# Attention steps 39 to 41 of the second chunk one step earlier, and seven scalings moved from VectorE to GpSimd

## The chip, the core and the metric

The program runs on one core of one Trainium2 chip. Its time is the device time of one execution in microseconds (us). The engines are named as in the profile: PE (TensorE, with PEld its weight loads), ACT (ScalarE), DVE (VectorE), POOL (GpSimd) and SP (SyncE, which here only issues DMAs). Each runs its own list of instructions in order; they wait for each other through semaphores.

## The reference

Top-32 attention over 4 batches, 8 heads, 576 positions and a head size of 64, then two feed-forward layers over 2304 tokens (512 to 2048 to 512). All data is fp32.

```python
scores = scale * np.matmul(q, k.transpose(0, 1, 3, 2))
kth = np.partition(scores, -top_k, axis=-1)[..., -top_k:-top_k + 1]
scores = np.where(scores >= kth, scores, -1000000000.0)
scores = scores - np.max(scores, axis=-1, keepdims=True)
attn = np.exp(scores)
attn = attn / (np.sum(attn, axis=-1, keepdims=True) + 1e-09)
x = np.matmul(attn, v)            # transposed and reshaped to (2304, 512)
h = x @ w_in                      # layer 0
x = np.maximum(0.01 * h, h) @ w_out
h = x @ w_in2                     # layer 1
g = np.where(h >= 1, h, np.where(h <= -1, 0.0, (h + 1) ** 2 / 4.0))
out = g @ w_out2
```

## The kernel before

**Attention.** Heads are taken in pairs. A group `gp` is one pair of heads of one batch with either the rows 0 to 255 or the rows 256 to 575. Each group is cut into items: two heads times 128 rows, which is two tiles of 128 x 576 scores, and for the last 64 rows of a batch a mixed item of one tile that holds 64 rows of each head. There are 144 tiles. A tile passes through these stations:

- PE makes the scores (L848, L849); ACT copies them out of PSUM (`copy_scores`, L1027).
- DVE finds the 32 largest of each row in four rounds: `top8` (MAX8, L1211) and, between the rounds, `drop8` (MATCH_REPLACE8, L1215).
- ACT masks (`keep`, L1046 and L1048) and exponentiates with a sum per row (`exponential`, L1056).
- DVE adds 1e-9 to the sums (`close_sum`, L1222) and inverts them (`invert_sum`, L1227).
- The probabilities are scaled by the inverse. ACT does an item's first tile (its `normalise`, L1062). The second tile is done by POOL (L726) for the items of the first chunk but the last, and by DVE (L1232) for all others.
- PE transposes both tiles into the PSUM tensor `ps_t`, with a remainder in `ps_av` (L864 to L871), ACT copies them to `p_t` and `p_rem` (L1069 to L1076), and after the last item of a group PE multiplies with V (`values`, L887, 20 products). ACT splits the result into a rounded high part and a raw copy (L1090, L1092), and POOL makes the low part (`low_x`, L732).

**Feed-forward.** The tokens are cut into seven chunks; the first is the 256 rows of groups 0 to 3 (items 0 to 7), the second the 320 rows of groups 4 to 7 (items 8 to 19). Work on a chunk is cut into units that write one PSUM bank of three: a hidden unit (H) has 4 sources, an output unit (O) 8 sources, and each source takes three products (high x high, low x high, high x low; L928, L929, L936). A unit of the first chunk is 12 or 24 products of 256 columns. In layer 1 a hidden unit is read twice by ACT (L1110, L1111), squared and clipped by DVE (L1238), joined by POOL (`join`, L747), rounded by ACT (L1123) and its low part made by POOL (`low_gate`, L741). ACT may not read a hidden unit before the low part of the third hidden unit back is made, and PE may not open a bank before ACT has read the unit three back. In the first chunk ACT (L1011) and POOL (L720) also split freshly loaded weights.

**The order of the work.** `make_plan` (L289) deals the units to steps 0 to 152, one step for each tile of attention, as far as a credit of `FILL` (4275 ns of PE work) a step goes; between the time when the first chunk's input is ready (`READY[0]`, step 21) and the second's (`READY[1]`, step 42) the credit is `FIRST_FILL`, the first chunk's work divided by the number of those steps. Each step's units come in three groups, and each engine writes its part of a step in a fixed order around them. `out_step` (L226) says in which step an item is scaled and transposed: 7 steps after its last tile, 6 for the last group of the second chunk (`hurried`, group 7, items 17, 18 and 19 with the tiles 31 to 35), 5 for the first chunk. In the steps from 21 on PE transposes an item between the second and the third group of units, and `values` of group 7 stands at the end of its step. In this kernel item 17 is transposed in step 38, item 18 in step 40 and item 19 in step 41, and the values product of group 7 ends step 41. DVE runs through tiles: its pass `t` makes the first two rounds of tile `t` and the last two of tile `t - 1`, with the units of step `t + 2` between them.

Around the change, PE's steps are, with S for the scores of an item, T for its transposes and V for a group's values product:

| step | units and attention work on PE |
|---|---|
| 35 | layer 1, block 0: H5, H6, H7 |
| 36 | S20; block 1: H0, H1; T15; H2 |
| 37 | H3; block 0: O0; T16 |
| 38 | O1; S21; V6; T17 |
| 39 | O2 |
| 40 | S22; O3; block 1: H4; T18 |
| 41 | H5; H6; T19; H7; V7 |
| 42 | second chunk, layer 0: H0; S23; H1 |

## Time and profile before

| | |
|---|---|
| median of 3 runs | 1165.05 us (1163.45 to 1166.36) |
| the profiled execution, own time | 1163.93 us |
| its span, first to last instruction | 1162.1 us |
| granted TensorE clock, mean | 0.979 of full |
| PE busy | 1092.6 us, 94% of the span |
| chain that ended last | PE 69%, DVE 18%, ACT 5%, issue 3%, POOL 3% |

The busy share says how full an engine is, the chain which engine's work was followed by the end, and the timelines and windows where the time is lost. In the timelines a duration often overlaps the start of the next instruction of the same engine. The clock is given as a share of full speed, 2.4 GHz; 0.5 is 1.2 GHz.

### The profile page before, as it was taken

Reading aid. Unit: us, or ns where it says so; the run is one execution under the profiler, and the core shown is the slowest. Engines: PE = TensorE matmul, PEld = TensorE weight load, DVE = VectorE, ACT = ScalarE, POOL = GpSimd, SP = SyncE. Lnnn points to the kernel's source line nnn. Section 1 sums busy time; section 2 is a strip of 40 time slices with the busy share of each in tenths; the row PEclk is TensorE's granted clock in tenths of the full one; section 3 lists DMA queues with packets and bytes.
Section 4 is the critical chain, followed back from the end, with each engine's and each line's share of the span. In section 5 each row is a group of like instructions: output and inputs, shape, how many; then the busy total and the mean of one; then the engine's idle time right before and its main releaser. Section 6 shows DMA issues by size and latency. Waiting matters only on the chain.

```text
span 1162.1 us, 21227 instructions
## 1 busy us (share of the span) xinstructions
PE 1092.6 (94%) x7568; PEld 1002.3 (86%) x7568; DVE 877.2 (75%) x1921; ACT 791.6 (68%) x1827; POOL 464.8 (40%) x493
## 2 busy tenths in 40 slices
PE   5457998899999999999999999999999999999998
PEld 3336887799988998899999879989998999999998
DVE  7999999889889998999979989888993005300234
ACT  7887999787788877887869868778885224322332
POOL 5654468552264432643225434225532234222322
PEclk9679999999999999999999999999999999999999
DMA  7988988697657788788667667565555677787764
GB/s 247 351 337 298 366 307 311 217 377 252 234 201 237 246 307 289 274 291 293 237 232 245 220 218 247 203 211 192 169 195 210 213 257 253 254 285 251 256 246 139
DMA packets 90680, 295.52 MB, mean 254 GB/s; under 512 B 10064, under 2 KB 13776, under 8 KB 90576
## 3 DMA queue, kind: packets, MB, share of 16 engines
q1 hardware_dynamic: 86544, 289.45, 71.2%
q10 hardware_dynamic: 4032, 4.72, 1.1%
q8 instruction: 61, 1.00, 0.3%
q14 instruction: 43, 0.35, 0.1%
HBM read 255.85 MB, written 38.27 MB: 253 GB/s over the span
## 4 chain that ended last, share of the span: by engine, by line
PE 69%; DVE 18%; ACT 5%; issue 3%; POOL 3%; DMA 1%; SPq 0%; POOLq 0%; ACTq 0%; DVEq 0%
PE ps_f L928 19%; PE ps_f L936 18%; PE ps_f L929 18%; DVE top L1211 8%; DVE work L1215 7%; PE ps_av L887 6%; PE ps_s L848 3%; PE ps_t L864 2%; DVE part_r L1238 2%; PE ps_t L870 2%; DMA raw<-wd 1%; PE ps_t L848 1%; POOL gate L741 1%; ACT probs L1056 1%; ACT probs L1048 1%
## 5 line engine op out<-in xcount | busy, mean ns | idle before, releaser
L1211 DVE MAX8 top<-work 128x8 f32<-128x576 f32 x432 | 310.2, 743 | 0.2
L928 PE MATMUL ps_f<-xy,w_ring 128*128 128x384 f32 (+2 forms) x896 | 289.3, 323 | 5.7 <-ACT gate L1115 2.0
L928 PE MATMUL ps_f<-gate,w_ring 128*128 128x384 f32 (+2 forms) x896 | 285.2, 318 | 0.0
L936 PE MATMUL ps_f<-gate,w_ring 128*128 128x384 f32 (+2 forms) x896 | 280.9, 314 | 4.1 <-POOL gate L741 4.0
L936 PE MATMUL ps_f<-xy,w_ring 128*128 128x384 f32 (+2 forms) x896 | 281.1, 314 | 1.6 <-POOL xy L751 1.1
L929 PE MATMUL ps_f<-xy,w_ring 128*128 128x384 f32 (+2 forms) x896 | 280.3, 313 | 0.0
L929 PE MATMUL ps_f<-gate,w_ring 128*128 128x384 f32 (+2 forms) x896 | 279.8, 312 | 0.0
L1215 DVE MATCH_REPLACE8 work<-top,work 128x576 f32<-128x576 f32 x288 | 213.3, 740 | 0.0
L741 POOL TENSOR_TENSOR gate<-part_r,gate 128x384 fp32r<-128x384 f32 (+2 forms) x112 | 101.3, 905 | 244.0 <-ACT gate L1115 243.9
L928 PEld LDWEIGHTS ps_f<-xy,w_ring 128*128 128x128 f32 x896 | 169.7, 189 | 19.9 <-issue 10.1
L928 PEld LDWEIGHTS ps_f<-gate,w_ring 128*128 128x128 f32 x896 | 169.2, 189 | 6.5 <-issue 6.2
L936 PEld LDWEIGHTS ps_f<-gate,w_ring 128*128 128x128 f32 x896 | 169.2, 189 | 6.4 <-POOL gate L741 6.4
L936 PEld LDWEIGHTS ps_f<-xy,w_ring 128*128 128x128 f32 x896 | 169.6, 189 | 3.1 <-POOL xy L751 1.9
L1246 DVE TENSOR_TENSOR y_acc<-ps_f,y_acc 128x384 f32<-128x384 f32 (+2 forms) x56 | 27.7, 494 | 189.7 <-PE ps_f L936 189.7
L929 PEld LDWEIGHTS ps_f<-xy,w_ring 128*128 128x128 f32 x896 | 169.9, 190 | 0.0
L929 PEld LDWEIGHTS ps_f<-gate,w_ring 128*128 128x128 f32 x896 | 169.3, 189 | 0.0
L741 POOL TENSOR_TENSOR gate<-part_o,gate 128x384 fp32r<-128x384 f32 (+2 forms) x112 | 103.8, 928 | 72.2 <-ACT gate L1123 71.8
L1238 DVE SCALAR_TENSOR_TENSOR part_r<-part_r 128x384 f32<-128x384 f32 (+2 forms) x112 | 69.9, 624 | 61.7 <-ACT part_o L1111 61.5
L1056 ACT ACTIVATE probs<-probs,shift 128x576 f32<-128x576 f32 x144 | 113.3, 787 | 0.8
L1048 ACT ACTIVATE probs<-scores,top 128x576 f32<-128x576 f32 x144 | 113.2, 786 | 0.0
L1211 DVE MAX8 top<-scores 128x8 f32<-128x576 f32 x144 | 107.8, 749 | 6.7 <-ACT scores L1020 6.7
L1215 DVE MATCH_REPLACE8 work<-top,scores 128x576 f32<-128x576 f32 x144 | 106.6, 740 | 0.0
(85 smaller groups left out, 1842.0 us busy)
## 6 DMA issues: line engine op xcount, KB each, us to landing
w_ring<-w_split SPq DMA_DIRECT2D x408, 512.0 KB, 4.2
w_split<-w_ring SPq DMA_DIRECT2D x40, 512.0 KB, 6.3
raw<-wd SPq DMA_DIRECT2D x64, 256.0 KB, 5.8
w_split<-xy SPq DMA_DIRECT2D x24, 512.0 KB, 5.0
v_sb<-vd SPq DMA_DIRECT2D x32, 320.0 KB, 5.7
kq<-kqd SPq DMA_DIRECT2D x16, 480.0 KB, 4.9
kq<-kqd SPq DMA_DIRECT2D x15, 416.0 KB, 3.6
out_t<-y_acc ACTq DMA_DIRECT2D x12, 192.0 KB, 4.3
```

The source lines that it names most:

```text
L741: pool.tensor_tensor(gate_of(u, 1), src[:, u.h % G_SLOTS, 0:u.width], gate_of(u, 0).bitcast(F32), ALU.subtract).then_inc(gate_low_done[u.l ...
L848: pe.matmul(out[:, 0, 0:PART], q[0:D, rows[0]], k[0:D, even:even + PART], start=start, stop=stop)
L887: mm = pe.matmul(ps_av[a * D:(a + 1) * D, 0:width], w, x, start=c == 0, stop=c == KC)
L928: pe.matmul(out, w[:, 0, m], high, start=first, stop=False)
L929: pe.matmul(out, w[:, 1, m], high, start=False, stop=False)
L936: mm = pe.matmul(out, w[:, 0, m], low, start=False, stop=end)
L1048: act.activation(probs[:, it.n % P_SLOTS, a * S:(a + 1) * S], scores[:, it.n % S_SLOTS, a, :], ACT.Prelu, bias=last, scale=-1.0, alpha=1.0 ...
L1056: act.activation(p, p, ACT.Exp, bias=shift[:, t % TOP_SLOTS:t % TOP_SLOTS + 1], scale=-STEEP, accum_out=row_sum[:, it.n % T_SLOTS, a:a + 1 ...
L1211: op = dve.max(top[:, t % TOP_SLOTS, 8 * r:8 * r + 8], source(t, r))
L1215: dve.match_replace(work[:, t % 2, :], top[:, t % TOP_SLOTS, 8 * r:8 * r + 8], source(t, r), LOWEST).then_inc(dve_step, 1)
L1238: dve.scalar_tensor_tensor(out=r, in0=r, scalar=1.0, in1=r, op0=ALU.min, op1=ALU.mult).then_inc(curved, 1)
L1246: dve.tensor_tensor(y_cols(u), bank(u), y_cols(u), ALU.add).then_inc(read_by_dve, 1)
```

## The change

1. `sooner` names the items 18 and 19. Their `out_step` is one earlier, 39 and 40, and with it the values product of group 7 (step 40). `READY[1]` becomes 41, so the first chunk's units are dealt over 20 steps instead of 21 (`FIRST_FILL` 3987 ns instead of 3797 ns), and every unit from there on stands one step earlier relative to the tiles. In step 152, after the last tile, 88 units are left instead of 90.
2. ACT scales items 18 and 19 in the step in which they are transposed, behind the exponential, instead of one step ahead. Tiles 32 to 35, in steps 36 to 39, are masked at the start of the step and exponentiated before the second group, instead of half a step later.
3. DVE has a written-out pass for tile 36 (`finish_second`), which finishes tile 35 first and closes item 18 inside; item 19 is closed earlier in the next pass.
4. `by_pool` now takes the second tiles of items 8, 9, 11, 12, 14, 15 and 17 from DVE to POOL. POOL does each at the start of the step ahead of the transposes.

The steps on PE become:

| step | units and attention work on PE |
|---|---|
| 35 | layer 1, block 0: H7; block 1: H0, H1 |
| 36 | S20; H2; H3; T15 |
| 37 | block 0: O0; O1; T16 |
| 38 | O2; S21; V6; T17 |
| 39 | O3; block 1: H4; T18 |
| 40 | H5; S22; H6; T19; H7; V7 |
| 41 | second chunk, layer 0: H0; H1 |

```diff
--- before.py
+++ after.py
@@ -223,8 +223,13 @@
     return gp == CHUNKS[1].last_gp
 
 
+def sooner(it):
+
+    return hurried(it.gp) and it.gp == ITEM_OF[it.first - 1].gp
+
+
 def out_step(it):
-    return it.last + (5 if starts_early(it.gp) else 6 if hurried(it.gp) else 7)
+    return it.last + (5 if starts_early(it.gp) or sooner(it) else 6 if hurried(it.gp) else 7)
 
 
 def values_step(gp):
@@ -232,6 +237,7 @@
     return out_step(last) + (not starts_early(gp) and not hurried(gp))
 
 
+SECOND_END = LAST_OF_GROUP[CHUNKS[1].last_gp]
 FIRST_END = LAST_OF_GROUP[CHUNKS[0].last_gp]
 READY = [values_step(c.last_gp) + 1 for c in CHUNKS]
 FIRST_NS = 2 * BLOCKS * PRODUCTS * (BLOCK_F * CK + CK * BLOCK_F) * (CHUNKS[0].width / 2.4 + 12)
@@ -476,7 +482,7 @@
 
 def by_pool(it):
 
-    return starts_early(it.gp) and it.last < FIRST_END
+    return it.gp <= CHUNKS[1].last_gp and not it.mixed and it.last != FIRST_END and not sooner(it)
 
 
 def by_dve(it):
@@ -788,8 +794,10 @@
                     low_direct(a)
 
             for s, (first, second, third) in enumerate(PLAN):
-                if s in OUT_AT and by_pool(OUT_AT[s]):
+                if s < READY[0] and s in OUT_AT and by_pool(OUT_AT[s]):
                     normalise(OUT_AT[s])
+                if s >= READY[0] and s + 1 in OUT_AT and by_pool(OUT_AT[s + 1]):
+                    normalise(OUT_AT[s + 1])
                 if s == READY[0] - 2:
                     low_x(CHUNKS[0].last_gp)
                 if s == READY[0] - 1:
@@ -1144,6 +1152,8 @@
 
             for s, (first, second, third) in enumerate(PLAN):
                 done, t, soon = OUT_AT.get(s), exp_tile(s), hurried_tile(s)
+                if t is None and s >= READY[0]:
+                    t, soon = soon, None
                 if s < READY[0]:
                     if done:
                         normalise(done)
@@ -1178,7 +1188,9 @@
                         copy_scores(it)
                 if t is not None:
                     exponential(t)
-                if s + 1 in OUT_AT:
+                if done and sooner(done):
+                    normalise(done)
+                if s + 1 in OUT_AT and not sooner(OUT_AT[s + 1]):
                     normalise(OUT_AT[s + 1])
                 if soon is not None:
                     keep(soon)
@@ -1265,16 +1277,48 @@
                 normalise(ITEM_OF[t - 1])
                 drop8(t, 1)
 
+            def finish_second(t, count, shut, first, second, third):
+
+                dve.wait_ge(dve_step, count)
+                top8(t - 1, 2)
...
+                dve.wait_ge(scores_copied, 2 * ITEM_OF[t].n + 2)
+                top8(t, 0)
+                close_sum(shut)
+                dve.wait_ge(dve_step, count + 3)
+                drop8(t, 0)
+                dve.wait_ge(dve_step, count + 4)
+                invert_sum(shut)
+                if by_dve(shut):
+                    normalise(shut)
+                dve.wait_ge(dve_step, count + 5)
+                top8(t, 1)
+                dve.wait_ge(dve_step, count + 6)
+                drop8(t, 1)
+
             for s in range(-VECTOR_AHEAD, len(PLAN)):
                 t = s + VECTOR_AHEAD
                 first, second, third = PLAN[t + VECTOR_AHEAD] if t + VECTOR_AHEAD < len(PLAN) else ((), (), ())
                 new, old = t < TILES, 0 < t <= TILES
                 shut = item_closing(t)
-                early = shut is not None and starts_early(shut.gp)
+                early = shut is not None and (starts_early(shut.gp) or shut.last == SECOND_END)
                 late = shut is not None and not early
                 before = count
                 if t == FIRST_END + 1:
                     finish_first(t, count)
+                    count += 7
+                    continue
+                if t == SECOND_END + 1:
+                    finish_second(t, count, shut, first, second, third)
                     count += 7
                     continue
                 if new:
```

Line numbers of the kernel after are 8 higher on PE and ACT, 6 on POOL and 12 on DVE. On ACT, from the exponential of tile 36 to the copy of item 19's transposes (the first row of the last copy is `p_t<-ps_t 128x4x2x64`), steps 40 and 41 read before:

```order
L1037 ACTIVATE kq_split<-kq 128x832
L1046 ACTIVATE shift<-top 128x1
L1048 ACTIVATE probs<-scores,top 128x576
L1110 ACTIVATE part_r<-ps_f 128x256
L1111 ACTIVATE part_o<-ps_f 128x256
L1011 ACTIVATE w_ring<-raw 128x512
L1056 ACTIVATE probs,row_sum<-probs,shift 128x576
L1123 ACTIVATE gate<-part_o 128x256
L1110 ACTIVATE part_r<-ps_f 128x256
L1111 ACTIVATE part_o<-ps_f 128x256
L1011 ACTIVATE w_ring<-raw 128x512
L1073 ACTIVATE p_t<-ps_t 128x4x2x64
```

And after, from the copy of item 18's transposes, in step 40:

```order
L1078 ACTIVATE p_rem<-ps_av 128x128
L1118 ACTIVATE part_r<-ps_f 128x256
L1119 ACTIVATE part_o<-ps_f 128x256
L1019 ACTIVATE w_ring<-raw 128x512
L1035 ACTIVATE scores<-ps_s 128x2x288
L1035 ACTIVATE scores<-ps_t 128x2x288
L1070 ACTIVATE probs<-probs,row_inv 128x576
L1131 ACTIVATE gate<-part_o 128x256
L1118 ACTIVATE part_r<-ps_f 128x256
L1119 ACTIVATE part_o<-ps_f 128x256
L1019 ACTIVATE w_ring<-raw 128x512
L1081 ACTIVATE p_t<-ps_t 128x4x2x64
```

The split of K and Q (L1037), the masking and the exponential of tile 36 no longer stand before the copy of item 19; the copy of the scores of item 22 (`scores`) and the scaling of item 19 (`probs<-probs,row_inv`) now do.

On DVE, the pass of tile 36 before, from its first `top8` to the scaling of item 18:

```order
L1211 MAX top<-scores 128x8
L1211 MAX top<-work 128x8
L1215 MATCH_REPLACE work<-top,scores 128x576
L1215 MATCH_REPLACE work<-top,work 128x576
L1211 MAX top<-work 128x8 x2
L1222 TENSOR_SCALAR row_eps<-row_sum 128x1 x2
L1215 MATCH_REPLACE work<-top,work 128x576
L1227 RECIPROCAL row_inv<-row_eps 128x2
L1232 TENSOR_SCALAR probs<-probs,row_inv 128x576
```

And after, from the third round of tile 35:

```order
L1223 MAX top<-work 128x8 x2
L1227 MATCH_REPLACE work<-top,work 128x576
L1223 MAX top<-work 128x8
L1227 MATCH_REPLACE work<-top,work 128x576
L1223 MAX top<-work 128x8
L1223 MAX top<-scores 128x8
L1234 TENSOR_SCALAR row_eps<-row_sum 128x1 x2
L1227 MATCH_REPLACE work<-top,scores 128x576
L1239 RECIPROCAL row_inv<-row_eps 128x2
L1244 TENSOR_SCALAR probs<-probs,row_inv 128x576
L1223 MAX top<-work 128x8
```

Tile 35's last two rounds now come first, with none of tile 36's work between them, and item 18's sum is closed after one round of tile 36 instead of after two.

On POOL, in the run of hidden units of layer 1 in steps 34 to 36, before (`part_o` is the join, `gate` the low part, `w_ring` a weight split):

```order
L741 TENSOR_TENSOR gate<-part_o,gate 128x256
L747 TENSOR_TENSOR part_o<-part_r,part_o 128x256
L741 TENSOR_TENSOR gate<-part_o,gate 128x256
L720 TENSOR_TENSOR w_ring<-raw,w_ring 128x512
L747 TENSOR_TENSOR part_o<-part_r,part_o 128x256
L741 TENSOR_TENSOR gate<-part_o,gate 128x256
L747 TENSOR_TENSOR part_o<-part_r,part_o 128x256
L741 TENSOR_TENSOR gate<-part_o,gate 128x256
```

And after:

```order
L753 TENSOR_TENSOR part_o<-part_r,part_o 128x256
L747 TENSOR_TENSOR gate<-part_o,gate 128x256
L726 TENSOR_TENSOR w_ring<-raw,w_ring 128x512
L732 TENSOR_TENSOR probs<-probs,row_inv 128x576
L753 TENSOR_TENSOR part_o<-part_r,part_o 128x256
L747 TENSOR_TENSOR gate<-part_o,gate 128x256
L753 TENSOR_TENSOR part_o<-part_r,part_o 128x256
L747 TENSOR_TENSOR gate<-part_o,gate 128x256
```

The scaling of item 15 (`probs`) now stands between the low part of one hidden unit and the join of the next; it waits for the inverse of DVE's pass for tile 32.

## Rows read from the trace of the kernel before

**Rows 1.** Page, part 1: busy time, share of the span, instructions.
```profile
PE 1092.6 (94%) x7568; PEld 1002.3 (86%) x7568; DVE 877.2 (75%) x1921; ACT 791.6 (68%) x1827; POOL 464.8 (40%) x493
```

**Rows 2.** Windows: from:to, length, busy (instructions) by engine, PEclk, DMA share, GB/s.
```profile
100.00:180.00 80.00, 76.71 (x606) 68.31 (x606) 77.55 (x175) 71.52 (x176) 48.95 (x52) 1.00 0.91 332
...
180.00:232.00 52.00, 42.87 (x329) 36.31 (x328) 47.63 (x108) 43.12 (x107) 33.62 (x38) 0.93 0.74 264
...
232.00:880.00 648.00, 638.51 (x4738) 584.33 (x4736) 595.85 (x1344) 510.97 (x1189) 257.77 (x286) 1.00 0.70 243
```

**Rows 3.** Timeline, PE: start, duration, instruction, [idle before it and releaser].
```profile
181.19 0.39 PE L928 MATMUL ps_f<-xy,w_ring 128*128 128x256 f32 x1 [0.42 <-ACT part_o L1111]
...
184.31 0.39 PE L928 MATMUL ps_f<-xy,w_ring 128*128 128x256 f32 x1 [1.42 <-ACT part_o L1111]
...
187.67 0.52 PE L864 MATMUL ps_t<-ident,probs 128*128 128x128 f32 x3 [1.67 <-issue]
...
199.89 0.37 PE L848 MATMUL ps_s<-kq_split 64*128 64x288 f32 x1 [1.76 <-ACT p_rem L1076]
...
206.37 0.63 PE L864 MATMUL ps_t<-ident,probs 128*128 128x128 f32 x4 [0.96 <-ACT x_raw L1092]
...
224.75 3.86 PE L887 MATMUL ps_av<-p_t,v_sb 128*64 128x320 f32 x16 [2.89 <-issue]
```

**Rows 4.** Timeline, PE: two neighbouring products of one unit.
```profile
190.00 0.28 PE L936 MATMUL ps_f<-xy,w_ring 128*128 128x256 f32 x1
190.12 0.28 PE L928 MATMUL ps_f<-xy,w_ring 128*128 128x256 f32 x1
```

**Rows 5.** Chain that ended last: start, us, what; values products, half and full clock.
```profile
201.22 4.21 PE ps_av L887 x20
...
224.75 4.40 PE ps_av L887 x20
...
367.36 2.84 PE ps_av L887 x20
```

**Rows 6.** Window in the values product of step 38, PE alone: busy, PEclk, DMA.
```profile
202.00:204.00 2.00, 2.00 (x10) 0.52 0.16 27
```

**Rows 7.** Timeline, ACT, steps 36 to 41.
```profile
186.22 0.70 ACT L1027 ACTIVATE scores<-ps_s 128x576 f32<-128x576 f32 x1
...
216.12 0.78 ACT L1062 ACTIVATE probs<-probs,row_inv 128x576 f32<-128x576 f32 x1 [1.22 <-DVE row_inv L1227]
...
218.91 0.92 ACT L1037 ACTIVATE kq_split<-kq 128x832 fp32r<-128x832 f32 x1
...
219.88 0.79 ACT L1048 ACTIVATE probs<-scores,top 128x576 f32<-128x576 f32 x1
...
221.60 0.81 ACT L1056 ACTIVATE probs<-probs,shift 128x576 f32<-128x576 f32 x1
...
223.71 0.65 ACT L1073 ACTIVATE p_t<-ps_t 128x512 f32<-128x512 f32 x1
```

**Rows 8.** Timeline, DVE: the close of item 18, and two squarings.
```profile
182.96 0.40 DVE L1238 SCALAR_TENSOR_TENSOR part_r<-part_r 128x256 f32<-128x256 f32 x1
...
197.81 1.22 DVE L1238 SCALAR_TENSOR_TENSOR part_r<-part_r 128x256 f32<-128x256 f32 x1
...
209.55 0.22 DVE L1222 TENSOR_SCALAR row_eps<-row_sum 128x1 f32<-128x1 f32 x2 [2.92 <-ACT probs L1056]
```

**Rows 9.** Timeline, POOL.
```profile
183.44 0.73 POOL L747 TENSOR_TENSOR part_o<-part_r,part_o 128x256 f32<-128x256 f32 x1 [2.05 <-DVE part_r L1238]
...
197.68 1.07 POOL L758 TENSOR_TENSOR kq_split<-kq,kq_split 128x416 fp32r<-128x416 f32 x1
```

**Rows 10.** Source lines 1232 and 726: count, min/median/max ns, first and last start.
```profile
L1232 DVE TENSOR_SCALAR probs<-probs,row_inv x57: 519/523/1276, 91.0 to 883.3; 128x576 f32<-128x576 f32 x57
...
L726 POOL TENSOR_TENSOR probs<-probs,row_inv x7: 1145/1146/1147, 24.3 to 84.6; 128x576 f32<-128x576 f32 x7
```

**Rows 11.** Chain that ended last: the values product at 682 us.
```profile
682.47 4.20 PE ps_av L887 x20
```

More of the change, by code:

```diff
@@ L1266, in finish_first @@
                 drop8(t, 1)
+            def finish_second(t, count, shut, first, second, third):
+                dve.wait_ge(dve_step, count)
+                top8(t - 1, 2)
+                for u in first:
+                    event(u)
+                dve.wait_ge(dve_step, count + 1)
+                drop8(t - 1, 2)
+                for u in second:
+                    event(u)
+                dve.wait_ge(dve_step, count + 2)
+                top8(t - 1, 3)
+                for u in third:
+                    event(u)
+                dve.wait_ge(scores_copied, 2 * ITEM_OF[t].n + 2)
[11 more added lines that the diff above has]
+                drop8(t, 1)
             for s in range(-VECTOR_AHEAD, len(PLAN)):
```

## The prediction

> **What bounds the kernel now.** I read the page's shares first: PE is busy 94% of the span [rows 1], so the time is PE's work, which the change leaves alone (the same units, scores, transposes and values products), plus what PE idles and what it runs at half clock. Then the busy time by stretch shows where that is [rows 2]: before 180 us PE misses 3.3 of 80 us, from 232 to 880 us 9.5 of 648 us, but from 180 to 232 us, which are steps 36 to 41, 9.1 of 52 us, at a mean clock of 0.93. That is the stretch that the change rewrites. Next PE's timeline there [rows 3]. Six waits make up the 9.1 us: 0.42 and 1.42 us for a bank that ACT had not read, 1.67 us ahead of the transposes of item 15, 1.76 us ahead of the scores of item 21 (ACT had not copied item 16's transposes), 0.96 us between V6 and the transposes of item 17, and 2.89 us ahead of V7. After the two long ones the clock was 0.5: V6 and V7 took 4.21 and 4.40 us, where the same product takes 2.84 us later on [rows 5], and inside V6 PE did 10 products in 2 us at a clock of 0.52 [rows 6]. So half clock costs 1.37 + 1.56 = 2.9 us. Waits and clock together are 12.0 us, the most that this stretch can give.
>
> Last I read who is late. In steps 33 to 38 ACT and DVE are: a product starts every 0.12 us [rows 4], so a hidden unit of 12 products takes PE 1.44 us, and ACT copied the scores of item 20 at 186.22 us [rows 7], over 5 us after PE had gone on to the hidden unit of 181.19 us [rows 3]. In steps 39 to 41 it is ACT's order: ahead of item 19's copy at 223.71 us stand the split of K and Q (0.92 us), the masking (0.79) and the exponential (0.81) of tile 36 [rows 7], 2.52 us that V7 does not need. DVE has 47.6 busy of 52 us here [rows 2]; its largest wait, 2.92 us, is for the exponential of tile 34 [rows 8].
>
> **The change part by part.**
>
> *The wait ahead of V7.* The 2.52 us of ACT work go behind V7. Item 19's scaling (0.78 us) and the scores of item 22 now stand ahead of T19, not between T19 and the copy, so behind T19 ACT only reads H6, splits a weight and copies. PE meanwhile does H7, 1.44 us. I put the wait at 0.4 us (bounds 0 and 2.9), a gain of 2.5.
>
> *New waits ahead of T18 and T19.* The step is packed: behind O3 ACT does an exponential and a scaling, 0.81 + 0.78 = 1.59 us, and reads the unit, while PE has only H4, 1.44 us: T18 waits some 0.3 us. Ahead of T19 ACT copies two halves of scores (0.70 each [rows 7]) and scales (0.78): 2.2 us, of which PE's H6 covers 1.44 and the first half overlaps the scores' own end: 0.5 us. Bounds for the two together: 0 (DVE and ACT come ahead) and 2.9 (each as bad as half the wait for V7 twice over); I take 0.8. The new DVE pass puts item 18's inverse earlier: tile 34's exponential now stands ahead of the copies of V6 and T17, so the 2.92 us wait should go, and DVE is not what T18 waits for. T19's inverse came 0.2 us before ACT's scaling at 216.12 us, after 1.22 us of ACT waiting [rows 7]; with DVE 2.92 us less late that wait goes too. If it does not, T19 is later by up to 1.2 us, inside the bounds.
>
> *The wait ahead of S21.* Before, H3, O0, T16, O1 gave ACT one output unit (24 products, 2.9 us) to catch up from the hidden units before T16. After, O0 and O1 stand ahead of T16: 2.9 us more of PE work that ACT hardly takes part in. The 1.76 us go (bounds: all or nothing).
>
> *The clock.* Half clock followed the waits of 1.76 and 2.89 us. It did not follow the waits up to 187.67 us, 3.5 us in sum. If the two shrink as above, I take both losses off: 1.37 + 1.56 = 2.9 us; the bounds are 2.9 and 0, since where a half-clock stretch falls is not in my hands.
>
> *The run of hidden units.* It now stands a little earlier and closer to the tiles: two more hidden units ahead of S20. The work of ACT in it is the same, so the 3.5 us of waits (0.42, 1.42, 1.67) stay. Into it falls the scaling of item 15 by POOL, 1.146 us [rows 10], which first waits for the inverse at the end of DVE's pass. Behind it in POOL's queue are joins and low parts, behind these ACT's rounding and reading, behind these PE's banks. POOL has idle time there (2.05 us of waiting for a squaring [rows 9]), and DVE comes earlier, since scalings of 0.52 us median [rows 10] left it: 4 before that place, 2.1 us. Bounds: minus 2.1 (DVE's lead reaches PE) and plus 3.2 (a whole 1.15 us and the 2.05 us wait added). Nearest to the row of POOL's own scaling: I take plus 1.2. The scalings of items 8, 9, 11 and 12 fall where PE has waits of 3.3 us in 80 and POOL is busy 49 of 80 us [rows 2]: nothing. Those of 14 and 17 stand ahead of V5 and of the three output units, which cover them: nothing. Item 18 stays on DVE.
>
> *V6 to T17*, 0.96 us, stays: nothing stands between them before or after. *The feed to the second chunk*: POOL makes the low part of group 7 right behind the last joins; I add 0.7 us for its lag, between 0 and 1.4, in a place where the split of K and Q no longer stands ahead of it. *DMAs*: the same list, V of group 11 one step sooner; the share of the DMA engines is 0.74 in the stretch [rows 2], and no wait of PE names them: nothing. *After step 41* every unit is a step sooner, two units fewer are behind the last tile; PE is bound there and its work the same: nothing.
>
> The sum: -2.5 + 0.8 - 1.8 - 2.9 + 1.2 + 0.7 = -4.5 us. DVE, relieved by seven scalings (3.7 us) and the 2.92 us wait, should also shorten the later DVE stretches a little, where V took 4.20 us at 682 us [rows 11] instead of 2.84; I take a third of that 1.4 us, 0.5. Together -5.0 us: 1163.93 for the profiled execution becomes 1158.9. That execution was 1.1 us under the median of the runs, so for the median I forecast 1165.05 - 5.0 = 1160.0 us.
>
> *A rule against it.* Of DVE's squarings, the one at 182.96 us took 0.40 us, and the one at 197.81 us, begun 0.13 us behind a POOL instruction of 1.07 us, took 1.22 us [rows 8, 9]. The Trainium skill says in "GPSIMD Engine Reference", Key points, that GpSimd shares its SBUF interfaces with VectorE, and that this hurts VectorE instructions in a two-port mode or with two SBUF inputs. The squaring has two inputs, and the trace agrees. By that rule the scalings of items 14, 15 and 17, the three in the layer 1 run, can each hold a squaring for 0.82 us more. If that reached PE in full, the sum would be -5.0 + 2.5 = -2.5 us instead of -5.0; by the rows DVE has shed more than this by then.
>
> **The rivals.**
>
> *A, given back later: no change.* DVE is in the chain for 18% of the span, and it is nearly as full as PE from 232 to 880 us, 596 to 639 us [rows 2]. If DVE's own queue sets when PE passes 682 us and the last tile, an earlier PE waits there for what it gained. For it: that fullness, and PE's waits are then on POOL and DVE work. Against: the plan puts one step more of units ahead of each tile, up to 4.3 us of PE work, so PE comes to a given tile only slightly earlier. Its price is 3 to 5 of the 5 us: 1163.5 us.
>
> *B, POOL in the loop: slower.* The place is steps 35 and 36. POOL waits for the inverse of item 15 ahead of joins that ACT and PE need. If the three-unit buffers are already used up there, as the waits of 0.42 and 1.42 us say, the wait (2.05 us as now on a squaring) plus 1.15 us goes straight to PE, and an idle time of 3.5 + 3.2 us draws one half-clock stretch (1.4 us): +4.6 against my +1.2. If the lag then also keeps S21 and V6 as they are, 3.1 us of gain are gone: -5.0 + 3.4 + 3.1 = +1.5 us, and a second scaling with the same price (item 14, 3.2 us, not covered by V5) makes it +4.7: 1169.7 us. It decides once POOL's wait for item 15's inverse is above 2 us. Against: DVE's lead of 2.1 us.
>
> *C, more than forecast.* The hidden run also loses its 3.5 us since DVE comes ahead, and T18 and T19 do not wait: -5.0 - 3.5 - 1.2 - 0.8 = -10.5: 1154.5 us.
>
> **How the numbers follow.** My forecast gets 0.48, C 0.12, A 0.25, B 0.15. About 0.3%, 3.5 us, is what a measurement of this kernel can tell from no change. Faster: C and most of the forecast (a sum under -3.5), 0.12 + 0.43. Same: A and the forecast's upper part, 0.25 + 0.05. Slower: B, 0.15. The forecast's own range is 1156 to 1163 us. The one given holds it, A, most of C and the milder end of B: 1154 to 1167.5 us.
>
> **What would show it.** Right: between the scores of item 20 and V7, PE's idle falls from 9 to about 6 us; S21 starts without a wait; the wait ahead of V7 is under 1 us; V6 and V7 take 2.8 to 3 us; DVE has no wait for the exponential of tile 34; waits of 0.2 to 1 us stand ahead of T18 and T19. Wrong: half clock in V6 or V7 all the same, which leaves up to 2.9 us of the gain; a wait of PE over 4 us in steps 35 and 36, with POOL idle ahead of a scaling (B); or PE idle after 232 us risen from 9.5 us in the 648 by several us (A).

## The result, and the profile after

The kernel after took 1158.56 us (median of 4 runs, 1156.76 to 1160.16) against 1164.62 us before (4 runs on the same chip). The ratio is 0.9951, with a 95% interval of 0.9939 to 0.9964: 5.7 us faster. The forecast was 1160.0 us and faster.

| | before | after |
|---|---|---|
| profiled execution, own time | 1163.93 us | 1158.78 us |
| its span | 1162.1 us | 1156.8 us |
| granted TensorE clock, mean | 0.979 | 0.987 |
| units behind the last tile | 90 | 88 |

Page of the kernel after: the busy shares, and the chain that ended last by engine.

```profile
PE 1092.0 (94%) x7568; PEld 1003.4 (87%) x7568; DVE 872.2 (75%) x1914; ACT 792.0 (68%) x1827; POOL 472.1 (41%) x500
...
PE 79%; DVE 8%; ACT 6%; POOL 2%; issue 2%; DMA 2%; SPq 0%; POOLq 0%; ACTq 0%; DVEq 0%
```

PE's work is as large as before [rows 1]. What changed is the chain: DVE fell from 18 to 8%, PE rose from 69 to 79%.

Windows of the kernel after, columns as in [rows 2]; the second ends 4 us sooner, since the program is ahead by then.

```profile
100.00:180.00 80.00, 75.22 (x587) 66.30 (x586) 72.91 (x168) 69.39 (x171) 52.08 (x55) 1.00 0.91 329
180.00:228.00 48.00, 41.48 (x335) 36.15 (x334) 43.29 (x98) 42.13 (x105) 35.79 (x40) 1.00 0.88 315
228.00:880.00 652.00, 643.50 (x4776) 592.31 (x4777) 601.29 (x1357) 514.76 (x1197) 259.68 (x288) 0.99 0.69 241
```

In the rewritten stretch PE misses 6.5 of 48 us where it missed 9.1 of 52, at full clock. Before 180 us it misses 4.8 us of 80 instead of 3.3, which the forecast did not have. From 228 us on it misses 8.5 of 652 (9.5 of 648 before).

PE's timeline of the kernel after, first at the boundary of layer 0 and layer 1, then in steps 36 to 41; columns as in [rows 3].

```profile
161.66 0.39 PE L936 MATMUL ps_f<-xy,w_ring 128*128 128x256 f32 x1 [0.22 <-ACT xy L1138]
162.47 0.39 PE L944 MATMUL ps_f<-xy,w_ring 128*128 128x256 f32 x1 [0.31 <-POOL xy L757]
165.26 0.39 PE L944 MATMUL ps_f<-xy,w_ring 128*128 128x256 f32 x1 [0.30 <-POOL xy L757]
...
184.04 0.39 PE L936 MATMUL ps_f<-xy,w_ring 128*128 128x256 f32 x1 [0.76 <-ACT part_o L1119]
189.55 0.39 PE L936 MATMUL ps_f<-xy,w_ring 128*128 128x256 f32 x1 [1.19 <-ACT part_o L1119]
192.91 0.63 PE L872 MATMUL ps_t<-ident,probs 128*128 128x128 f32 x4 [1.66 <-issue]
204.44 0.36 PE L856 MATMUL ps_s<-kq_split 64*128 64x288 f32 x1 [1.08 <-POOL kq_split L764]
209.29 0.63 PE L872 MATMUL ps_t<-ident,probs 128*128 128x128 f32 x4 [0.96 <-ACT x_raw L1100]
215.22 0.66 PE L872 MATMUL ps_t<-ident,probs 128*128 128x128 f32 x4 [0.46 <-ACT probs L1070]
220.87 0.66 PE L872 MATMUL ps_t<-ident,probs 128*128 128x128 f32 x4 [0.38 <-ACT probs L1070]
223.09 2.37 PE L895 MATMUL ps_av<-p_t,v_sb 128*64 128x320 f32 x16
225.93 0.41 PE L936 MATMUL ps_f<-xy,w_ring 128*128 128x320 f32 x1
...
898.29 2.37 PE L895 MATMUL ps_av<-p_t,v_sb 128*64 128x320 f32 x16
```

The wait ahead of V7 is gone (2.89 before), and V7 takes 2.84 us from 223.09 to 225.93 instead of 4.33 us. S21 still waits 1.08 us (1.76 before). T18 and T19 wait 0.46 and 0.38 us. The second chunk's first unit starts at 225.93 us. The last values product starts at 898.29 us.

The timeline of the kernel before at these last two places:

```profile
229.08 0.41 PE L928 MATMUL ps_f<-xy,w_ring 128*128 128x320 f32 x1
...
899.45 2.37 PE L887 MATMUL ps_av<-p_t,v_sb 128*64 128x320 f32 x16
```

So PE is 3.15 us ahead at the second chunk and only 1.16 us ahead at the last values product. Between the last values product and the end lie 1162.1 - 899.45 = 262.65 us before and 1156.8 - 898.29 = 258.51 us after: 4.1 us less, the two units that are no longer there. The 5.3 us of the two spans are these 1.16 + 4.14 us. These are single executions: in a second one of the kernel after (a1 below) the last values product starts at 902.64 us. So a difference of a few us between positions in two executions is not yet an effect; below, the weight lies on waits, on stretches within one execution and on the ratios.

DVE's timeline of the kernel after, where item 18 is closed:

```profile
207.56 0.22 DVE L1234 TENSOR_SCALAR row_eps<-row_sum 128x1 f32<-128x1 f32 x2 [0.18 <-ACT probs L1064]
...
208.61 0.52 DVE L1244 TENSOR_SCALAR probs<-probs,row_inv 128x576 f32<-128x576 f32 x1
```

The wait for the exponential fell from 2.92 us [rows 8] to 0.18 us, and item 18's second tile is scaled by 209.13 us, six us before T18.

### The profile page after: what moved, and what is told of

It is laid out like the page before. It is cut to its first block, busy times and chain, and to the rows that moved or that the text cites. A ratio compares the mean times of both kernels' runs of the same rounds, so it can differ in the third digit from the quotient of the medians.

```text
span 1156.8 us, 21227 instructions
## 1 busy us (share of the span) xinstructions
PE 1092.0 (94%) x7568; PEld 1003.4 (87%) x7568; DVE 872.2 (75%) x1914; ACT 792.0 (68%) x1827; POOL 472.1 (41%) x500
## 4 chain that ended last, share of the span: by engine, by line
PE 79%; DVE 8%; ACT 6%; POOL 2%; issue 2%; DMA 2%; SPq 0%; POOLq 0%; ACTq 0%; DVEq 0%
PE ps_f L936 21%; PE ps_f L944 20%; PE ps_f L937 20%; PE ps_av L895 7%; DVE top L1223 4%; DVE work L1227 3%; PE ps_s L856 3%; PE ps_t L872 2%; PE ps_t L878 2%; PE ps_t L856 1%; DMA raw<-wd 1%; DVE part_r L1250 1%; ACT probs L1064 1%; POOL gate L747 1%; ACT scores L1035 1%
## 5 line engine op out<-in xcount | busy, mean ns | idle before, releaser
L1250 DVE SCALAR_TENSOR_TENSOR part_r<-part_r 128x384 f32<-128x384 f32 (+2 forms) x112 | 69.7, 623 | 64.1 <-ACT part_o L1119 64.0
```

Of the source, the lines that this page charges most:

```text
L1250: dve.scalar_tensor_tensor(out=r, in0=r, scalar=1.0, in1=r, op0=ALU.min, op1=ALU.mult).then_inc(curved, 1)
```

## The experiments

All ran in 5 rounds beside the kernel before. Profiles of one kernel differ with where half clock falls: of the kernel after, one spans 1156.8 us and one 1161.2 us, with the waits of steps 35 to 41 equal within 0.03 us. So verdicts go by the ratios, and profiles are read for waits.

| run | median, us | ratio to before, 95% |
|---|---|---|
| a1_after_again | 1158.82 | 0.9959 (0.9944 to 0.9974) |
| e1_pool_only | 1165.62 | 1.0013 (1.0003 to 1.0023) |
| e2_order_only | 1158.31 | 0.9950 (0.9936 to 0.9965) |
| e4_both_groups | 1158.29 | 0.9952 (0.9938 to 0.9965) |
| e5_exp36_behind | 1165.09 | 1.0009 (1.0000 to 1.0018) |
| e6_plain_pass | 1160.24 | 0.9966 (0.9952 to 0.9980) |
| e7_masks_late | 1159.63 | 0.9955 (0.9943 to 0.9967) |
| e9_kq_behind | 1159.12 | 0.9954 (0.9942 to 0.9967) |
| e10_lead_only | 1162.03 | 0.9975 (0.9966 to 0.9985) |
| e11_no_lead | 1161.98 | 0.9982 (0.9972 to 0.9992) |
| e12_v7_path | 1164.77 | 1.0000 (0.9991 to 1.0009) |
| e13_two_leads | 1163.15 | 0.9993 (0.9985 to 1.0002) |

### The two parts: scalings alone, order alone

*a1_after_again* is the kernel after, timed again.

> The changed kernel once more, beside the others of this call, as their yardstick. From its first runs: ratio 0.995 to the kernel before, about 1158.6 us. Both theories expect that again, within 1.5 us.

*e1_pool_only*: the kernel before with the seven scalings on POOL, at the start of the step ahead of the transposes, and nothing else.

```diff
-    return starts_early(it.gp) and it.last < FIRST_END
+    return it.gp <= CHUNKS[1].last_gp and not it.mixed and it.last != FIRST_END and it.n != 18
...
```

> The kernel before with the seven scalings alone moved from VectorE to GpSimd (items 8, 9, 11, 12, 14, 15, 17), plan and steps as before. Theory W (the gain is that of PE's waits around S21 and V7 and of the half clock behind them, which the order brings): within 1.5 us of the kernel before, with the 2.89 us wait ahead of V7 and the half clock still there. Rival D (VectorE's relief is what brings it, as its share of the chain, 18% before and 8% after, suggests): 3 to 5 us faster.

*e2_order_only*: the kernel after with all seven back on DVE.

```diff
-    return it.gp <= CHUNKS[1].last_gp and not it.mixed and it.last != FIRST_END and not sooner(it)
+    return starts_early(it.gp) and it.last < FIRST_END
```

> The changed kernel with the seven scalings back on VectorE, order and steps as changed. Theory W: 4 to 6 us faster than the kernel before, as the whole change is. Rival D: within 1.5 us of the kernel before. If VectorE's lead is needed for the tight order (both together), it comes out between, 1 to 3 us faster, with waits ahead of T18 and T19 that grew by what VectorE is late.

The scalings alone make it slower by 0.13% (0.03 to 0.23), 1.5 us, and without them the order and its plan have the whole gain, as far as intervals of some 1.6 us to either side can tell. PE's timeline of the kernel with the scalings alone:

```profile
184.66 0.39 PE L930 MATMUL ps_f<-xy,w_ring 128*128 128x256 f32 x1 [1.84 <-ACT part_o L1113]
...
200.44 0.58 PE L850 MATMUL ps_s<-kq_split 64*128 64x288 f32 x1 [1.97 <-ACT p_rem L1078]
```

1.84 us stood at 1.42 and 1.97 at 1.76 in [rows 3]; the other waits of this stretch are the same within 0.02 us. That fits POOL in the loop of the hidden units, at +0.6 us; where the other 0.9 us of the 1.5 lie is not shown. In the new order the scalings cost PE as much or more: the waits in the run of hidden units (columns as above, 184 to 193 us) are 3.61 us in the kernel after and 1.02 + 1.67 = 2.69 us in e2. With the regrouped steps of the next section they are 3.99 us with the scalings on POOL (e4) and 3.07 us with them on DVE (e13). Both pairs differ by 0.92 us, which is too little for the ratios to tell.

### The groups of steps 29 and 32

The layer boundary at 160 to 166 us loses 0.9 us on PE (busy 5.10 of 6.00 us) where the kernel before loses next to nothing (its PE is busy 19.93 of 20.00 us from 160 to 180 us). In *e4_both_groups* the second group of the units of steps 29 and 32 is emptied into the third, so that they stand on the other side of the transposes.

```diff
+        if s in (29, 32):
+            second = first
```

> The changed kernel with two steps' groups cut otherwise: in step 29 the first output unit of block 1 stands behind the transposes of item 11 and not ahead of them, and in step 32 the transposes of item 13 stand ahead of layer 1's first hidden unit and not behind it. Theory L (the changed plan loses 2 us at the boundary of the layers, since VectorE, blocked 4.36 us on that output unit, adds the last output unit late, and no transposes cover it): VectorE's wait of 4.36 us and PE's small waits at layer 1's first two units go, and it is 1 to 2 us faster than the changed kernel, near 1157 us. Rival: PE is held by ACT and GpSimd in the run of hidden units right behind anyway, where it waits 3.6 us, so the 2 us come back there: no change against the changed kernel, within 1 us.

In its profile only one wait of 0.31 us is left at the boundary, and V7 starts at 221.52 us instead of 223.09. Of this 1.57 us, 1.0 us stands already at the transposes near 115 us (114.72 against 115.72), ahead of the regrouped steps. From there to the values product V5 the boundary gives 1.3 us, and 0.75 us of it is lost again by V7. The time is the kernel after's: 0.9952 and 0.9951. A gain of 1 us would not show in these intervals, so it is not shown whether the remaining 0.6 us reach the end.

### The wait ahead of V7 by itself

*e5_exp36_behind*: the kernel before with ACT's masking and exponential of tile 36 moved behind V7's copy.

```diff
+                behind = t if s == READY[1] - 1 else None
+                t = None if behind is not None else t
...
+                if behind is not None:
+                    keep(behind)
+                    exponential(behind)
```

> The kernel before with one thing moved: ACT masks and exponentiates tile 36 behind the copy of V7 in step 41, instead of ahead of item 19's copy (1.6 us of its work). The plan, the steps and the scalings stay. Theory W (each wait of PE in this stretch reaches the end of the kernel): the wait ahead of V7 falls from 2.89 to about 1.2 us, half clock in V7 becomes rarer, and it is 1.5 to 3 us faster than the kernel before. Rival A (given back later): under 1 us.

PE's timeline of this kernel, then POOL's:

```profile
223.80 2.37 PE L887 MATMUL ps_av<-p_t,v_sb 128*64 128x320 f32 x16 [1.28 <-issue]
...
230.84 0.42 PE L936 MATMUL ps_f<-xy,w_ring 128*128 128x320 f32 x1 [2.32 <-POOL xy L732]
```

```profile
228.69 1.27 POOL L720 TENSOR_TENSOR w_ring<-raw,w_ring 128x512 fp32r<-128x512 f32 x1
229.92 0.87 POOL L732 TENSOR_TENSOR xy<-x_raw,xy 128x320 fp32r<-128x320 f32 x1
```

The wait fell by 1.6 us and V7 ran at full clock, worth 3.1 us together, and nothing came out at the end. From the second chunk's first unit to 560 us PE now misses 6.6 us, where it missed 4.3 in the kernel before; the difference is the one new wait. POOL makes the low part of group 7 (L732) at 229.92 us, where before it was 230.03: its queue of weight splits, joins and low parts was already full up to there. PE now waits 2.32 us for it, and the clock is 0.63 of full right behind, in this window:

```profile
232.00:235.00 3.00, 3.00 (x16) 2.83 (x15) 1.52 (x6) 2.72 (x7) 3.00 (x4) 0.63 0.72 212
```

*e12_v7_path* also moves the first half of the split of K and Q, 1.07 us of that queue, behind the low part.

```diff
-                if s in KQ_LOWERED_AT:
+                if s in KQ_LOWERED_AT and s != READY[1] - 1:
                     low_kq(KQ_LOWERED_AT[s], 0)
...
+                    if s == READY[1] - 1:
+                        low_kq(KQ_LOWERED_AT[s], 0)
```

> The kernel before with tile 36's mask and exponential on ACT behind the copy of V7, as in an earlier run, and GpSimd's first half of the split of K and Q for group 10 behind the low part of group 7. In that earlier run the wait ahead of V7 fell from 2.89 to 1.28 us, but 2.32 us of waiting for the low part came up in the second chunk's first unit. Theory W with GpSimd's queue as the last link: the half goes out of that queue, the wait for the low part falls to 1.2 us or less, and it is 1 to 3 us faster than the kernel before. Rival: GpSimd's joins and weight splits alone hold the low part, and nothing is won: within 1 us.

Its ratio is 1.0000. PE's and POOL's timelines:

```profile
231.99 0.42 PE L938 MATMUL ps_f<-xy,w_ring 128*128 128x320 f32 x1 [2.07 <-POOL xy L732]
```

```profile
225.46 0.73 POOL L747 TENSOR_TENSOR part_o<-part_r,part_o 128x256 f32<-128x256 f32 x1 [1.14 <-DVE part_r L1245]
...
231.08 0.86 POOL L732 TENSOR_TENSOR xy<-x_raw,xy 128x320 fp32r<-128x320 f32 x1
```

The shorter queue starts later, since a join waits 1.14 us for DVE's squaring, and PE meets it again with 2.07 us.

### Pieces of the order

*e6_plain_pass*: the kernel after without the written-out pass for tile 36.

```diff
-                if t == SECOND_END + 1:
-                    finish_second(t, count, shut, first, second, third)
-                    count += 7
-                    continue
```

> The changed kernel without VectorE's written-out pass for tile 36; item 18 is closed, inverted and scaled at the end of the ordinary pass. Everything else as changed. Theory: VectorE finished item 18's scaling at 209.1 us in the trace of the changed kernel, while T18 started at 215.2 us, so there are 6 us of slack against some 2 us that the ordinary pass is later: no change against the changed kernel, within 1 us. Rival: the tight order needs the pass: T18 waits, 1 to 3 us slower than the changed kernel.

*e7_masks_late*: the kernel after with tiles 32 to 35 masked half a step later, as before.

```diff
-                if t is None and s >= READY[0]:
-                    t, soon = soon, None
```

> The changed kernel with tiles 32 to 35 masked and exponentiated at their old places, half a step later, the steps as changed. Theory W: ACT then has the exponential of tile 35 behind item 18's copy and the one of tile 34 behind V6, so item 18's sum closes 3 to 5 us later, T18 waits 2 to 3 us instead of 0.46, half clock comes back in some executions, and it is 2 to 4 us slower than the changed kernel. Rival: ACT only shifts the same work about and PE's waits are the same in sum: within 1 us.

*e9_kq_behind*: e4_both_groups with ACT's split of K and Q (0.98 us) behind item 16's copy, for which S21 waits.

```diff
+                if s == READY[1] - 4:
+                    high_kq(KQ_LOWERED_AT[s])
...
-                if s + 1 in KQ_LOWERED_AT:
+                if s + 1 in KQ_LOWERED_AT and s != READY[1] - 5:
```

> The kernel with the two regrouped steps (29 and 32), and in it ACT's split of K and Q for group 9 (0.9 us) put behind the copy of item 16's transposes, where it stood ahead of it. Theory W: S21's wait of 1.07 us falls to 0.2 us, and it is about 1 us faster than with the regrouped steps alone, 5.5 to 7.5 us faster than the kernel before. Rival: GpSimd, whose half of that split is late by as much, holds weight splits and low parts behind it, and PE waits there instead: no gain over the regrouped steps.

None of the three differs from the kernel after beyond its interval, so Theory W is not borne out in e7 or e9. e6's waits are the same; its ratio is the highest, and whether the pass brings the 1.7 us between the medians stays open. In e9 the wait ahead of S21 only fell from 1.07 to 0.78 us; S21 starts there at 204.87 us, ahead of POOL's half of the split for group 9 (205.73 us), so it does not need that half. e7 trades one wait for another; its PE timeline:

```profile
203.41 0.36 PE L856 MATMUL ps_s<-kq_split 64*128 64x288 f32 x1 [0.17 <-ACT p_rem L1084]
...
220.02 0.66 PE L872 MATMUL ps_t<-ident,probs 128*128 128x128 f32 x4 [0.80 <-ACT probs L1070]
228.11 0.42 PE L944 MATMUL ps_f<-xy,w_ring 128*128 128x320 f32 x1 [1.14 <-POOL xy L738]
```

S21 is nearly free of its wait, T19 waits 0.80 us, and the second chunk again stands behind the low part of group 7, 1.14 us.

### The order around V7 against the lead over the tiles

After the change the plan also has a step's worth of units more ahead of each later tile. *e10_lead_only* gives the kernel before this lead and nothing else: the plan from step 45 on is the kernel after's, with 88 units left.

```diff
-        credit += FILL if s >= READY[1] else FIRST_FILL
+        credit += (2 * FILL if s == 44 else FILL) if s >= READY[1] else FIRST_FILL
```

> The kernel before with nothing changed in steps 0 to 43 and one step's credit more at step 44, so that from step 45 on every feed-forward unit stands where the changed kernel has it, one step earlier, and 88 units are left for the last step instead of 90. Theory W (PE is the bound there; only waits removed count): within 1.5 us of the kernel before. Rival P (the pace of the tiles is set by VectorE, so each unit dealt ahead of them is won; the changed kernel's values products stand at the same times as before, and 4.1 us less are left behind the last tile): 3 to 5 us faster.

*e11_no_lead* takes it from the kernel after, 90 units left.

```diff
-        credit += FILL if s >= READY[1] else FIRST_FILL
+        credit += (0 if s == 44 else FILL) if s >= READY[1] else FIRST_FILL
```

> The changed kernel with no credit at step 44, so that from step 45 on every unit stands where the kernel before has it (90 left at the end), while steps 21 to 43 are as changed. Theory W: 3 to 5 us faster than the kernel before, since the waits around S21 and V7 are gone all the same. Rival P: within 1.5 us of the kernel before.

The lead alone: 0.9975, 2.9 us (1.7 to 4.0). The order alone: 0.9982, 2.1 us (0.9 to 3.3). Their sum is 5.0 us, and the whole is 5.7 (4.8 when timed again). Neither theory is borne out as it stands: the first value is just under the 3 to 5 us of Rival P, the second lies between the two. The kernel with the lead alone still has the wait ahead of V7, 2.88 us. The timeline at the last values product, of the kernel with the lead alone, then of the one without it:

```profile
901.73 2.38 PE L887 MATMUL ps_av<-p_t,v_sb 128*64 128x320 f32 x16
```

```profile
898.26 2.37 PE L895 MATMUL ps_av<-p_t,v_sb 128*64 128x320 f32 x16
```

From the second chunk's first unit to the last values product the kernel before takes 670.4 us and the one with the lead alone 672.0 us, with 4.1 us more of units done. The kernel after takes 672.4 us, and without the lead (e11) it takes 672.9 us; the eight profiles of kernels with one step of lead lie between 671.3 and 674.2 us. So most of the 4.1 us of units costs no time there, and behind the last tile all of it is saved. PE's waits between tiles show where they went. Windows from the second chunk's first unit to 560 us, of the kernel before, then of the one with the lead alone:

```profile
229.08:560.00 330.92, 326.66 (x2585) 300.69 (x2584) 306.63 (x699) 261.24 (x618) 135.50 (x156) 1.00 0.78 269
```

```profile
229.75:560.00 330.25, 328.35 (x2608) 304.06 (x2607) 303.11 (x696) 263.43 (x623) 138.39 (x159) 1.00 0.79 274
```

And PE's waits of over 0.5 us in them, again before and with the lead alone:

```profile
331.75 0.37 PE L848 MATMUL ps_s<-kq_split 64*128 64x288 f32 x1 [1.29 <-ACT p_rem L1070]
...
348.55 0.36 PE L848 MATMUL ps_s<-kq_split 64*128 64x288 f32 x1 [0.53 <-ACT p_rem L1070]
...
353.98 0.63 PE L864 MATMUL ps_t<-ident,probs 128*128 128x128 f32 x4 [0.66 <-issue]
```

```profile
325.97 0.37 PE L848 MATMUL ps_s<-kq_split 64*128 64x288 f32 x1 [0.93 <-ACT p_rem L1070]
...
479.33 0.63 PE L864 MATMUL ps_t<-ident,probs 128*128 128x128 f32 x4 [0.69 <-issue]
```

PE misses 4.3 us there before and 1.9 us with the lead; the kernel after and a1 miss 1.9 us too. From 560 us to the last values product it misses 1.2 us more with the lead (6.5 against 5.2), so 1.1 us of idle time is won in all. The rest of the 2.9 us is not located in these traces.

The kernel without the lead is not the order alone in every respect: no unit is left for its step 44, and it has two waits that neither the kernel before nor the one after has.

```profile
241.96 0.63 PE L872 MATMUL ps_t<-ident,probs 128*128 128x128 f32 x4 [1.04 <-issue]
...
252.96 0.41 PE L936 MATMUL ps_f<-xy,w_ring 128*128 128x320 f32 x1 [1.15 <-DVE y_acc L1258]
```

So the order's 2.1 us may be too low by up to these 2.2 us. Against it the kernel after is faster by 3.6 us, by the two ratios, where the lead alone gave 2.9.

In the chain DVE has 12% with the lead alone and 14% with the order alone, 4 to 6 points less than the 18% before. But it has 15% in e1 too, which is slower: the share alone does not tell a gain.

### A second step of lead

*e13_two_leads* has e4's regrouped steps, the scalings on DVE as in e2, and a second step's credit at step 45: 86 units left.

```diff
-        credit += FILL if s >= READY[1] else FIRST_FILL
+        credit += (2 * FILL if s == 45 else FILL) if s >= READY[1] else FIRST_FILL
```

> The kernel after the change with the scalings back on VectorE, the two groups of steps 29 and 32 regrouped as in the run e4_both_groups, and a second step's worth of fillers moved ahead: at step 45 the plan's credit grows by 2 * FILL, so that 86 output and product units instead of 88 are left behind the last tile's values. Nothing of the computation is left out. Theory L (a unit moved from behind the last tile to a place between tiles is worth time as long as VectorE still stands in the chain of waits, 8 to 9 per cent of it after the change): the second lead moves another 4.1 us of TensorE's work ahead, and pays less than the first one's 2.6 to 2.9 us: 0.5 to 2 us, so 1156.5 to 1158 us beside the 1158.3 us of e2_order_only and e4_both_groups. Rival M (the tiles from step 45 on are by now paced by TensorE itself, 94 per cent busy): within 0.5 us of 1158.3 us. Rival N: with less work left behind the last tile VectorE's last output units end the kernel later, 1159 us or more.

Theory L fell: 1163.15 us, 4.8 us over e2 and e4. Rival N has the sign, not the place. The loss is not at the end but between the tiles. PE's timeline, with its last values product, and a window around the wait:

```profile
340.81 0.37 PE L858 MATMUL ps_s<-kq_split 64*128 64x288 f32 x1 [3.04 <-ACT p_rem L1080]
...
907.13 2.37 PE L897 MATMUL ps_av<-p_t,v_sb 128*64 128x320 f32 x16
```

```profile
336.00:346.00 10.00, 6.96 (x46) 4.70 (x45) 9.96 (x22) 9.58 (x23) 6.87 (x8) 0.83 0.50 169
```

DVE's timeline of the same kernel:

```profile
277.51 0.22 DVE L1236 TENSOR_SCALAR row_eps<-row_sum 128x1 f32<-128x1 f32 x2 [5.47 <-ACT probs L1066]
```

The last values product is 10.0 us later than in e2 (897.12 us), more than the 4.4 us by which two executions of one kernel differed. Of it 4.1 us are the units moved ahead. In the stretch between, PE misses 12.2 us where it misses 8.7 in e2, and its busy time is longer by 1.9 us beyond the units, as work at half clock would make it. By the traces, the second lead brings PE later to each item's scores (the values product of group 8 starts at 265.5 us, 259.2 in e2), and DVE runs dry for 5.47 us at 277 us, where e2's largest wait for an exponential between 230 and 360 us is 1.17 us. PE then waits 3.04 us at 340.81 and falls below full clock. That the one wait brings on the other is argued, not shown. The two edits that e13 has beside the credit were each run with the kernel after's time, but not together; 0.5 us of the 10 already stand at the second chunk's first unit (226.33 against e2's 225.83).

## Why the prediction was right, and where its steps were not

The time (1158.6 for 1160.0 us) and the sign were right. That the amount is so close is partly luck: about half of it came by the road forecast (2.1 us by e11, a little more if its own two waits are counted), the other half by a term priced at nothing. What was taken too high at V7 and S21 was made up by what was left out after step 41.

- *The wait ahead of V7*, -2.5: it went in full (-2.89), as said. But what it is worth was mis-sized. By itself it hid the wait for POOL's queue to the low part of group 7 (e5, e12: no gain). In the kernel after that queue moved too: POOL's low part came at 226.90 instead of 230.03 us, with half of the split of K and Q no longer ahead (POOL's timeline, of after and of before):

```profile
226.90 0.88 POOL L738 TENSOR_TENSOR xy<-x_raw,xy 128x320 fp32r<-128x320 f32 x1 [0.43 <-ACT x_raw L1100]
```

```profile
230.03 0.88 POOL L732 TENSOR_TENSOR xy<-x_raw,xy 128x320 fp32r<-128x320 f32 x1
```

The forecast said that this split leaves the place, and made the place cost +0.7 us all the same; no wait of PE stands there in the kernel after. It should have asked of it first how early V7 may come at all.
- *New waits ahead of T18 and T19*, +0.8: 0.46 + 0.38 = 0.84.
- *The wait ahead of S21*, -1.8: -0.68. The step that failed is "the 1.76 us go". The output units did relieve ACT, but the split of K and Q, a masking, an exponential and a scaling still stand between the copies of items 15 and 16, as ACT's timeline after shows, and e7 (masks later) brings the wait to 0.17 us. POOL's half of the split, the releaser that the profile names, ends at about the same time (203.30 us and 1.06), but it is not the cause. In e2 it ends 1.0 us ahead of S21 and the wait is 1.08 us all the same, put down to ACT; in e9 S21 starts ahead of it.

```profile
198.09 0.98 ACT L1045 ACTIVATE kq_split<-kq 128x832 fp32r<-128x832 f32 x1
...
199.06 0.85 ACT L1056 ACTIVATE probs<-scores,top 128x576 f32<-128x576 f32 x1
...
200.81 0.85 ACT L1064 ACTIVATE probs<-probs,shift 128x576 f32<-128x576 f32 x1
...
201.58 0.84 ACT L1070 ACTIVATE probs<-probs,row_inv 128x576 f32<-128x576 f32 x1
...
203.34 0.67 ACT L1081 ACTIVATE p_t<-ps_t 128x512 f32<-128x512 f32 x1
```

- *The clock*, -2.9: V6 and V7 run at full clock, as said.
- *The run of hidden units*, +1.2: its waits are 0.76, 1.19 and 1.66, 3.61 us against 3.51. Two parts hide in this. "The 3.5 us of waits stay" did not hold: in the new order without the scalings on POOL they are 2.69 us (e2). With them they are 0.92 us more, near the +1.2. POOL did not wait for item 15's inverse (186.00 us), but 0.97 us for item 17's (199.54 us).
- *The rule weighed there*, a squaring held up by POOL, would have made the sum -2.5. The contention that the Trainium skill names ("GPSIMD Engine Reference", Key points) did not grow by the scalings: the 112 squarings take 69.9 us in all in the kernel before and 69.7 us both in e1 and in the kernel after. So e1's +1.5 us does not come that way.
- *Before step 36* nothing was priced. The first chunk's units dealt over 20 steps instead of 21 cost some 1 us at the layer boundary. e4 takes that back, with no gain that its ratio can tell.
- *After step 41*, "nothing" and 0.5 for DVE's later stretches: this was the large miss. The lead is worth 2.9 us by itself (e10). The forecast held that PE is bound there and its work the same. But PE is not bound at every tile; a unit put between tiles fills in part time that PE otherwise loses there (the waits at 332, 349 and 354 us), and is then missing behind the last tile, where PE does nothing but units. 88 instead of 90 units stood in the text as a fact with no price.
- *The scalings' relief*: said to be worth little directly, and no gain of it is seen (e2 against the kernel after, each within some 1.6 us).

Rival A, given back later, holds for one part: what V7 gains alone is given back within 8 us, at the low part. It named DVE; there the engine is POOL, and one of the two new waits of e11 is put down to DVE. Rival B's mechanism fits e1 and e2 at 0.6 to 0.9 us, a seventh to a fifth of its 4.6 us, without the wait for item 15's inverse that it asked for. C did not come.

## What to carry to other kernels

A wait is worth what lies between it and the next late thing: before pricing one, look up when the following consumer's own input (here a 0.9 us GpSimd instruction behind a full queue) was ready. Where fillers are dealt between paced work, how far ahead they are dealt has a best value: with DVE at 18% of the chain one step paid 2.9 us, at 7 to 9% a second one cost 4.8. Two points are no rule, and the share by itself misled in e1, so try one step each way and do not extrapolate. Moving work from VectorE to an idler GpSimd was no gain here, where GpSimd sits in a loop that PE waits for.

## What the runs showed of the hardware

Half clock did not follow the length of the wait. The transposes near 115 us wait 3.34 us in the kernel after, 3.32 us in its second execution (a1) and 2.24 us in e2. A window right behind each, in this order:

```profile
116.00:118.00 2.00, 2.00 (x20) 2.00 (x19) 2.00 (x5) 1.98 (x6) 1.18 (x2) 1.00 1.02 410
```

```profile
117.00:119.00 2.00, 2.00 (x16) 2.00 (x15) 2.00 (x5) 1.98 (x6) 1.19 (x2) 0.73 1.04 416
```

```profile
115.00:117.00 2.00, 2.00 (x12) 2.00 (x11) 2.00 (x5) 1.98 (x6) 0.73 (x1) 0.50 1.05 420
```

Behind the longest wait PE did 20 instructions in 2 us at 2.4 GHz, behind the shortest 12 at 1.2 GHz, and the same kernel with the same wait did 16, part of them at the lower level. The same kernel's two profiles are 4.4 us apart in span. In a forecast, a term for the clock is therefore a chance and not a sum.
